# Two head pairs in one slot beside the hidden layer, and two more weight pieces split by VectorE

## The reference

```
scores = (q @ k.T) / sqrt(64)                 # 4 batches x 12 heads, 448 rows each, float32
attn   = exp(cap * tanh(scores / cap))        # the reference subtracts the row maximum first
attn   = attn / (attn.sum(-1) + 1e-9)
x      = attn @ v                             # heads side by side: 1792 x 768
h      = x @ w_in                             # 768 x 2048
g      = s * relu(h)**2 + b
out    = g @ w_out                            # 2048 x 768
```

## Time and profile before

| what | value |
|---|---|
| runs | 593.20, 591.67, 592.83 us (median 592.83) |
| the profiled execution | 592.27 us, its span 590.5 us |
| PE busy, PE weight loads busy | 99%, 79% |
| VectorE, ScalarE, GpSimd busy | 73%, 58%, 31% |
| mean busy share of the DMA engines | 58.3% (queue 1) |
| granted TensorE clock | full in all 40 slices |

### The profile page before, as it was taken

How to read it: one execution, slowest core, us unless ns; L and a number is a source line. 1 busy time by engine, 2 the same in 40 slices (tenths; PEclk the granted TensorE clock), 3 DMA queues, 4 the chain that set the end, 5 groups by cost and what they waited for, 6 DMA issues and landing times.

```text
span 590.5 us, 8848 instructions
## 1 busy us (share of the span) xinstructions
PE 584.9 (99%) x3080; PEld 469.4 (79%) x3080; DVE 430.9 (73%) x646; ACT 342.0 (58%) x409; POOL 182.3 (31%) x143
## 2 busy tenths in 40 slices
PE   8999999999999999999999999999999999999997
PEld 4335778668868777878777999999999999999997
DVE  4898999978677768769774235578878999775453
ACT  7995775775575676666752456545456445543330
POOL 0113976403434343434334333141333333000000
PEclk9999999999999999999999999999999999999999
DMA  8342345343555546454444978978768799854532
GB/s 285 135 135 85 120 149 166 125 132 149 189 199 189 197 161 224 163 214 179 177 173 155 334 246 298 320 247 289 232 239 293 240 321 333 273 173 125 174 109 92
DMA packets 61611, 118.65 MB, mean 201 GB/s; under 512 B 6464, under 2 KB 44160, under 8 KB 61568
## 3 DMA queue, kind: packets, MB, share of 16 engines
q1 hardware_dynamic: 61568, 118.09, 58.3%
HBM read 78.75 MB, written 39.32 MB: 200 GB/s over the span
## 4 chain that ended last, share of the span: by engine, by line
PE 95%; ACT 2%; DVE 2%; issue 1%; POOL 0%; DVEq 0%; ACTq 0%
PE banks L780 14%; PE banks L782 13%; PE banks L781 13%; PE banks L820 12%; PE banks L819 12%; PE banks L818 12%; PE banks L719 9%; PE banks L675 6%; PE banks L743 2%; PE banks L618 1%; PE banks L699 1%; PE banks L838 1%; PE banks L754 0%; ACT e L1000 0%; DVE e_sum L1114 0%
## 5 line engine op out<-in xcount | busy, mean ns | idle before, releaser
L780 PE MATMUL banks<-x_hi,w_hi 128*128 128x448 f32 x384 | 142.6, 371 | 0.0
L782 PE MATMUL banks<-x_hi,w_lo 128*128 128x448 f32 x384 | 140.3, 365 | 0.0
L781 PE MATMUL banks<-x_lo,w_hi 128*128 128x448 f32 x384 | 140.3, 365 | 0.0
L819 PE MATMUL banks<-x_lo,w_hi 128*128 128x448 f32 x336 | 122.7, 365 | 0.0
L818 PE MATMUL banks<-x_hi,w_hi 128*128 128x448 f32 x336 | 122.7, 365 | 0.0
L820 PE MATMUL banks<-x_hi,w_lo 128*128 128x448 f32 x336 | 122.7, 365 | 0.0
L1007 ACT ACTIVATE hidden_sb<-banks 128x448 f32<-128x448 f32 x56 | 30.6, 546 | 100.2 <-PE banks L782 100.2
L780 PEld LDWEIGHTS banks<-x_hi,w_hi 128*128 128x128 f32 x384 | 72.1, 188 | 20.3 <-issue 14.8
L1025 ACT ACTIVATE x_hi<-e,beside 128x448 fp32r<-128x448 f32 x64 | 48.8, 763 | 49.9 <-PE banks L820 49.8
L782 PEld LDWEIGHTS banks<-x_hi,w_lo 128*128 128x128 f32 x384 | 72.1, 188 | 6.0
L781 PEld LDWEIGHTS banks<-x_lo,w_hi 128*128 128x128 f32 x384 | 72.1, 188 | 5.5
(11 more groups left out here) (138 smaller groups left out, 800.0 us busy)
## 6 DMA issues: line engine op xcount, KB each, us to landing
t_scratch<-work SPq DMA_DIRECT2D x32, 448.0 KB, 3.5
e<-t_scratch SPq DMA_DIRECT2D x64, 224.0 KB, 3.8
hidden_scratch<-hidden_sb SPq DMA_DIRECT2D x56, 224.0 KB, 1.9
work<-hidden_scratch SPq DMA_DIRECT2D x24, 448.0 KB, 4.1
e<-hidden_scratch SPq DMA_DIRECT2D x48, 224.0 KB, 4.3
beside<-q_k SPq DMA_DIRECT2D x23, 448.0 KB, 4.6
work<-w_out SPq DMA_DIRECT2D x16, 384.0 KB, 3.6
s_scratch<-work SPq DMA_DIRECT2D x16, 384.0 KB, 2.9
```

The costliest lines, as they stand in the source:

```text
L780: nc.tensor.matmul(out, w_hi[:, j, w], x_hi[:, batch % 2, c, :], start=c == 0, stop=False)
L781: nc.tensor.matmul(out, w_hi[:, j, w], x_lo[:, batch % 2, c, :], start=False, stop=False)
L782: last = nc.tensor.matmul(out, w_lo[:, j, w], x_hi[:, batch % 2, c, :], start=False, stop=c == CT - 1)
L819: nc.tensor.matmul(out, w_tile(w_hi_flat, i, k, d), ring(x_lo, n), start=False, stop=False)
```

## The change

1. The middle stage goes by quads: one slot for two pairs. In slot `quad` PE computes the scores of pair 2 quad + 2, the values of both pairs of the quad, their tails, the next quad's tail scores (now in banks 4 and 5), the scores of pair 2 quad + 3 (third tile in the value banks 6 and 7), and then the hidden tiles of two former slots. The last quad has no scores left; its two pairs are taken one by one, with three hidden tiles between them.
2. `FIRST_ENDS` and `ENDS` have three numbers: 4, 4 and 3 tiles beside batch 1, then 5, 5 and 6. Five tiles (`AHEAD`) and not two come ahead of the first slot; the scores of pair 7 stand between tiles 1 and 2.
3. `SPLIT` is 8: pair 7's scores are plain float32, and no halves are made of its q and k.
4. Pieces 6 and 7 of w_in are split by VectorE (`w_in_more`), ahead of the sums of pair 6, with semaphores of their own.
5. VectorE scales both pairs of a quad first and splits them after (`scale_two`; odd pairs use the buffer `turned`).
6. SyncE's and ScalarE's lists follow. The loads of pieces 10 to 13 now stand behind the first two stores of hidden tiles; the sums for the output layer go by two in a slot.

```diff
+MORE = 2
 EARLY = 2
-FIRST_ENDS = (4, 6, 9, 11, 13, 16)
-ENDS = (3, 5, 8, 11, 13, 16)
+AHEAD = 5
+FIRST_ENDS = (9, 13, 16)
+ENDS = (5, 10, 16)
+ALONE = 3
-SPLIT = PAIRS + 1
+SPLIT = PAIRS + 2
-COMBINE = PAIRS + 4
+COMBINE = QUADS + 1
...
 # SyncE: a piece's place is free
-                    sp.wait_ge(w_in_lo, piece - CT + 1 if piece < CT + 4 else piece - 3)
+                    if piece < CT + 4:
+                        sp.wait_ge(w_in_lo, piece - CT + 1)
+                    elif piece < CT + 4 + MORE:
+                        sp.wait_ge(w_in_more_lo, piece - CT - 3)
+                    else:
+                        sp.wait_ge(w_in_lo, nth_piece(piece - 4) + 1)
...
 # TensorE
+            def free_for_last(p):
+                if p % 2:
+                    pe.wait_ge(x_done, p - 1)
+                else:
+                    batch, tiles = tiles_beside(p // 2 - 1)
+                    pe.wait_ge(relu_done, batch * JT + tiles.start)
...
+            for quad in range(QUADS, B * QUADS):
+                p = 2 * quad
+                follows = quad + 1 < B * QUADS
+                if follows:
+                    scores_of(p + 2)
+                batch, tiles = tiles_beside(quad)
                 values(p)
+                if not follows:
+                    for j in tiles[:ALONE]:
+                        for c in range(CT):
+                            hidden_chunk(batch, CT * j + c)
+                    tiles = tiles[ALONE:]
+                values(p + 1)
+                tail_values(p, 2)
+                if follows:
+                    pe.wait_ge(last_read, last_group(p + 2))
+                    tail_scores(quad + 1, G1)
+                    scores_of(p + 3)
+                for j in tiles:
+                    for c in range(CT):
+                        hidden_chunk(batch, CT * j + c)
...
 # ScalarE
+                if SPLIT <= p + 4 < ALL:
+                    split_high(p + 4)
+                if follows:
+                    first_tanh(p + 2)
+                    last_tanh(p + 2)
+                    tails_tanh(p + 2)
+                    exponential(p + 2, 0)
+                    exponential(p + 2, 1)
+                    first_tanh(p + 3)
+                    last_tanh(p + 3)
+                rectify(batch * JT + tiles[0])
+                if follows:
+                    exponential(p + 3, 0)
+                    exponential(p + 3, 1)
+                rectify(batch * JT + tiles[1])
+                if SPLIT <= p + 5 < ALL:
+                    split_high(p + 5)
+                for j in tiles[2:]:
+                    rectify(batch * JT + j)
...
 # VectorE
-            split_low(SPLIT)
+            for n in range(MORE):
+                w_in_more(n)
             add_last_e(PAIRS)
+            split_low(PAIRS + 2)
+            sums_of(PAIRS + 1)
             invert(PAIRS)
+            invert(PAIRS + 1)
...
+                if SPLIT <= p + 3 < ALL:
+                    split_low(p + 3)
+                scale_two(p)
+                if SPLIT <= p + 4 < ALL:
+                    split_low(p + 4)
+                if follows:
+                    sums_of(p + 2)
+                if follows:
+                    invert(p + 2)
+                if follows:
+                    sums_of(p + 3)
+                if follows:
+                    invert(p + 3)
```

More of the change, by code:

```diff
@@ L268, in tails_group, with tiles_beside, slot_of @@
             return (p - PAIRS) // 2
[L270 to L278, removed]
+        def tiles_beside(quad):
+            batch, c = divmod(quad, QUADS)
+            ends = FIRST_ENDS if batch == 1 else ENDS
+            first = AHEAD if batch == 1 else 0
+            return batch - 1, range(ends[c - 1] if c else first, ends[c])
+        def slot_of(batch, j):
+            for quad in range((batch + 1) * QUADS, min((batch + 2) * QUADS, B * QUADS - 1)):
+                if tiles_beside(quad)[1].start == j:
+                    return quad
+            return None
         def stays(n):
@@ L544, in _ @@
                         load_w_in(piece)
[L546 to L563, removed]
+            load_qk(PAIRS + 3)
@@ new lines, in _ @@
+            for j in range(EARLY):
+                store_hidden(j)
+            for piece in range(CT + 4, CT + 8):
+                load_w_in(piece)
+            load_v(PAIRS + 2)
+            load_qk(PAIRS + 4)
+            for j in range(EARLY, AHEAD):
+                store_hidden(j)
+                for piece in range(CT + 8 + 2 * (j - EARLY), CT + 10 + 2 * (j - EARLY)):
+                    load_w_in(piece)
+            combined = 0
+            for quad in range(QUADS, B * QUADS):
+                batch, tiles = tiles_beside(quad)
+                for p in (2 * quad + 3, 2 * quad + 4):
+                    if p < ALL:
+                        load_v(p)
+                for p in (2 * quad + 5, 2 * quad + 6):
+                    if p < ALL:
+                        load_qk(p)
+                if quad > COMBINE and quad != COMBINE + 2:
+                    combine_load(combined)
+                for j in tiles:
+                    store_hidden(batch * JT + j)
+                    if quad > COMBINE and j == tiles[0]:
+                        combine_store(combined)
+                        combined += 1
+                    if quad >= COMBINE and j == tiles[-1 if quad == COMBINE + 1 else 1]:
+                        combine_load(combined)
+                    if quad >= COMBINE and quad != COMBINE + 1 and j == tiles[-1]:
+                        combine_store(combined)
+                        combined += 1
+                    if quad == QUADS:
+                        nth = CT + 14 + 2 * (j - AHEAD)
+                        for piece in range(nth, min(nth + 2, PIECES)):
+                            load_w_in(piece)
@@ L571, in _ @@
                 load_g(n)
-            combined = ALL - COMBINE - 1
             for j in range(JT):
@@ L765, in hidden_chunk @@
                     pe.wait_ge(last_read, last_group(PAIRS - 1))
[L766 to L768 removed]
+                if c == 0 and slot_of(batch, j) is not None:
+                    pe.wait_ge(tails_read, tails_group(2 * slot_of(batch, j) + 2))
                 if n == 0:
@@ L1050, in _ @@
                 exponential(p, 0)
-                if p == PAIRS:
-                    split_high(SPLIT)
                 last_tanh(p)
                 exponential(p, 1)
+            split_high(PAIRS + 2)
             for j in range(EARLY):
                 rectify(j)
[L1058 to L1070, removed]
+            first_tanh(PAIRS + 1)
+            last_tanh(PAIRS + 1)
+            exponential(PAIRS + 1, 0)
+            exponential(PAIRS + 1, 1)
+            for j in range(EARLY, AHEAD):
+                rectify(j)
+            split_high(PAIRS + 3)
+            for quad in range(QUADS, B * QUADS):
+                p = 2 * quad
+                follows = quad + 1 < B * QUADS
+                batch, tiles = tiles_beside(quad)
+                if SPLIT <= p + 4 < ALL:
[17 more added lines that the diff above has]
+                    rectify(batch * JT + j)
             for j in range(JT):
@@ L1345, in _ @@
             pool.wait_ge(x_hi_done, PAIRS)
-            for piece in range(CT, CT + 4):
+            for piece in range(CT + MORE, CT + 4):
                 high(piece)
-            for piece in range(CT, CT + 4):
+            for piece in range(CT + MORE, CT + 4):
                 low(piece)
```

123 lines of the change are left out of this document (66 added, 57 removed).

## The result

The changed kernel takes 596.41 us in the median of 16 runs, the kernel before 592.48 in 16 runs on the same chip: a ratio of 1.0072, interval 1.006 to 1.0085, 0.7% slower. Its runs lie between 593.9 and 603.0, those of before within 1.5 us; the ratio leaves out the two longest, 602.9 and 603.0, which lie over 1.5% above its fastest. The prediction was 591.5 with a range of 589.8 to 594.6. The profiled execution took 596.35, its span is 594.6 us, 4.1 more than before.

A forecast was written before the change was run, and what follows sets the result against it. PE, busy 99% of the span and without notable waits in the middle stage, was taken as the bound. Terms: -2.1 + 0.7 + 0.2 + 0.2 = -1.0 us, giving 591.5 us, range 589.8 to 594.6.

The forecast's parts named there:

- PE's stream, -2.1: PE's middle stage: fewer changes of kind save 1.4 and 1.2 us, pair 7's plain scores cost 0.5; together -2.1 us.
- The join: Second pair's values directly behind the first's on PE pay only their steps, 0.15 us less a run, 1.2 in all.
- the plain scores of pair 7: Pair 7's scores on PE as plain products, not split: about 2.6 us, 0.5 more than before.
- Tile 4's wait, 0.7: PE reaches hidden tile 4 at 70.6, w_in piece 11 is ready at 71.3: a wait of 0.7 us, bounds 0 and 5.1.
- The landing: Time for w_in loads to arrive before GpSimd's work for tile 4: taken as 3.0 us, from 2.8 to 5.5.
- tile 4 waits long: Rival: PE waits 2.5 to 5.1 us at tile 4, by late loads or slowed GpSimd; 594.5 us, chance 0.13.
- Tail scores, 0.2: Tail scores in each of eight slots may wait for `last_tanh` to empty their banks: 0.2 us in all, ends 0 and 0.8.
- VectorE, 0.2: VectorE's work per quad may outlast PE's first slot or three-tile slot: 0.2 us for both, ends 0 and 7.0.
- the bound that I gave as a rival: Rival: VectorE becomes the bound in the slots beside batch 1; 594.8 us, chance 0.12.

The follow-up runs named there:

- e1: The changed kernel with the loads of w_in pieces 10 and 11 issued ahead of the stores of hidden tiles 0 and 1: 590.60 us, ratio 0.9975.
- e9: The changed kernel with 8 extra products on PE, their result overwritten, ahead of hidden tile 4's wait for w_in: 594.01 us, ratio 1.0025.
- e3: The changed kernel with 15 extra products on PE, their result overwritten, ahead of hidden tile 4's wait for w_in: 594.94 us, ratio 1.005.
- e4: The changed kernel without the two pieces of w_in on VectorE, GpSimd doing pieces 6 to 23: 595.50 us, ratio 1.0059.
- e2: The changed kernel with four hidden tiles ahead of the first slot and five in it (AHEAD = 4): 593.65 us, ratio 1.0036.
- e5: The changed kernel with loads of pieces 10 and 11 ahead of the stores and no w_in pieces on VectorE: 595.85 us, ratio 1.0058.

## Why the prediction was wrong

*PE's stream, -2.1: right in its parts, and 0.3 to 0.5 too large.* From pair 7's first scores product to the first product of the output layer it is 322.25 us before (60.70 to 382.95) and 320.65 in e1 (60.61 to 381.26), 1.6 less. The join saves what was said (4.66 against 4.65 worked out), the plain scores of pair 7 take 2.45 where I had 2.6. The difference lies in single runs of hidden products that go at 0.2067 a step and not at 0.2027, from their first step to their last. Before, three runs of 36, 54 and 54 steps do that, 0.13 to 0.2 us each; in e1 runs of 72, 54, 108 and 54 steps, 1.1 us together. In the changed kernel it is three runs, 72, 108 and 54 steps: its stretch is 326.43 us (60.60 to 387.03), less the 6.02 lost at tile 4 320.41, 1.8 less than before. Longer runs lose more when they fall into it. What decides it is open; in e9 the slower step begins behind the wait, in the middle of a run.

*Tile 4's wait, 0.7: this is the step that failed.* The mechanism was the one named, and the measured delay of 3.15 us lies inside the bounds of 0 and 5.1. Two sizes were off. The landing took 3.90 where I took 3.0 (the four loads stand behind two stores and ahead of v, q and k, and the DMA share is 0.97 in that stretch; what made it longer was not separated). GpSimd took 6.3 for two pieces where I took 4.9. The prediction had VectorE idle beside the first piece and busy beside the second; as piece 10 came only at 67.12, VectorE's additions from 67.03 on lay beside the first one and the cast of the second. The longer durations are in the earlier trace rows; I chose near the short ones twice in a row for terms that add up. The rival *tile 4 waits long*, with its 0.13, is what came, for both reasons that it gives, the second on three of the four instructions.

*The half clock, 2.87: missing altogether.* My bound for that wait counted only the waiting, and so did the rival. In the kernel before PE never stood still for more than 0.5 us after its start, so no row showed what 3 us cost, and the sum had no term for it. With 3.15 us of waiting alone the profiled execution would have taken 596.35 - 2.87 = 593.5, in the range. The profiled executions of e3 and e9, with full clock, took 594.0. The 2.87 is the size in that execution; the same standstill cost 1.4 in the profiled one of e4 (15.70 less the 11.15 needed and less 3.12 of delay, 70.51 to 73.63), and the sixteen runs have mean clocks from 0.994 to 0.999. The clock does not order these runs: the seven with 0.997 go from 595.5 to 600.8 us.

*Tail scores, 0.2: nothing was lost.* The weight loads of the tail scores wait for `last_tanh` (L1015), 3.3 us in eight slots, but the tail scores start 0.80 behind the tail values as before: the loads wait in time that the array spends on the tail values.

```profile
PEld banks L758 <- ACT e L1015: 3.3, 8, 0.4
```

*VectorE, 0.2: nothing was lost, but with no room in the first slot.* e2 shows the bound that I gave as a rival: one tile less ahead of the first slot and PE waits 2.3 us. In e1, where PE is not late, the low half of pair 9 ends at 82.50, the scores that need it could start at 81.69 + 0.86 = 82.55 and start at 82.60. The changed kernel has room there only because of its 6 us at tile 4.

```profile
81.37 1.13 DVE L1267 TENSOR_TENSOR qk_lo<-beside,qk_hi 128x896 fp32r<-128x896 f32 x1
```

*What was lost in all:* -1.8 for the stream, + 3.15 + 2.87 at tile 4 is +4.2; the stretch from pair 7 to the output layer is 326.43 against 322.25, 4.2 longer, and the spans differ by 4.1. This holds for the profiled execution. That it took as long as the median of the sixteen is partly luck, since their spread is mostly unexplained.

## What to carry to other kernels

When work is moved ahead of a wait that nobody felt before, follow the whole chain behind the wait back to the queue entry that starts it, and place that entry by its new due time; where two causes end at the same moment, remove both or neither. Price a standstill of an otherwise full PE at more than its length: here 3.0 us of idle time brought 2.87 more by the half clock in one execution and 1.4 in another, while 1.3 us brought nothing. Idle time of an engine read from a kernel that stalls is no reserve, since the stall may have made it.

## What was not expected of the hardware

- The granted clock fell to 0.50 while PE stood still: 2.3 to 2.4 us after its last product in the three profiled executions with 3.0 us of idle time. It came back after 6.8 us in two of them (the changed kernel and e5) and after 3.4 in the third (e4), with PE at work without a gap since the wait. After a standstill of 2.3 us it fell for 3.4 us in the profiled execution of e2; three of e2's eight runs have a mean clock of 0.996 or 0.997, the other five 1.000. After 1.3 us in e9 all eight runs have 1.000.
- The changed kernel's sixteen runs spread over 9 us, with a mean clock between 0.994 and 0.999. The kernels whose PE idles for 1.3 us or less at tile 4 and behind it spread over 1.1 to 2.2 us, with one exception: e3, whose wait is filled, spreads over 5.0. Some of the long runs (600.8 at 0.997; 599.5 in e2 and 597.7 in e3 at 1.000) are not explained by the clock alone; no trace of one was taken.
